# The scores of two heads in the two halves of TensorE's array, all heads of a chunk in one block

## The reference

```
for t in range(768):                       # for each batch and head
    m_new  = max(f[t] + m, i[t])
    f_s, i_s = exp(f[t] + m - m_new), exp(i[t] - m_new);  m = m_new
    C = f_s * C + i_s * outer(v[t], k[t])  # 40 x 40
    n = f_s * n + i_s * k[t]
    y[t] = sigmoid(o[t]) * (C @ q[t]) / max(|n @ q[t]|, 1)
x  = y, heads side by side                 # (2, 768, 320)
h  = relu(x @ w_in);  u, v = halves of h   # 512 columns each
x  = (u * (w_spatial @ normalised(v) + b)) @ w_out
xk, xr = mixes of x and x one token earlier
out = sigmoid(xr @ w_r) * (relu(xk @ w_k) ** 2 @ w_v)
```

## Time and profile before

| | |
|---|---|
| median of 3 runs | 311.3 us (309.66 to 312.32) |
| the profiled execution's own time | 309.62 us |
| its span, first to last instruction | 307.9 us |
| TensorE busy, matmuls | 297.3 us |
| VectorE, ScalarE, GpSimd busy | 208.1, 168.1, 68.8 us |
| mean granted clock of TensorE | 0.994 of full speed |

### The profile page before, as it was taken

How to read it: one execution, slowest core, us unless ns; L and a number is a source line. 1 busy time by engine, 2 the same in 40 slices (tenths; PEclk the granted TensorE clock), 3 DMA queues, 4 the chain that set the end, 5 groups by cost and what they waited for, 6 DMA issues and landing times.

```text
span 307.9 us, 5430 instructions
## 1 busy us (share of the span) xinstructions
PE 297.3 (97%) x1908; PEld 285.5 (93%) x1908; DVE 208.1 (68%) x443; ACT 168.1 (55%) x369; POOL 68.8 (22%) x92
## 2 busy tenths in 40 slices
PE   7998979999999999999999999999999999999996
PEld 3997969988999898899999999998999999999996
DVE  7986889979878779726424887878873377555111
ACT  5778796865546355513124676699682458255000
POOL 8325436324444413621111201400000000000000
PEclk9999997999999999999999999999999999999999
DMA  4959942554166054000060020320001000100011
GB/s 108 262 188 287 336 139 68 156 165 147 44 228 177 12 202 142 0 0 2 0 191 15 0 66 1 94 80 0 0 2 43 24 0 1 45 21 0 26 61 43
DMA packets 12778, 25.99 MB, mean 84 GB/s; under 512 B 2000, under 2 KB 5552, under 8 KB 12752
## 3 DMA queue, kind: packets, MB, share of 16 engines
q1 hardware_dynamic: 12752, 25.65, 26.5%
HBM read 23.63 MB, written 2.02 MB: 83 GB/s over the span
## 4 chain that ended last, share of the span: by engine, by line
PE 65%; DVE 13%; ACT 9%; issue 6%; DMA 3%; POOL 1%; DVEq 0%; SPq 0%; ACTq 0%; POOLq 0%
PE ps_e L1202 12%; PE ps_s L1202 10%; PE ps_v L1202 9%; PE ps_in L1202 6%; PE ps_out L1202 6%; PE ps_t L1202 6%; PE ps_z L1202 4%; PE ps_in L1282 4%; PE ps_s L1273 4%; PE ps_out L1292 2%; DVE shifted L1113 2%; DMA mb<-maxima 1%; DMA maxima<-mx 1%; PE ps_z L1301 1%; DVE mixb L1136 1%
## 5 line engine op out<-in xcount | busy, mean ns | idle before, releaser
L1273 PE MATMUL ps_s<-qkt 128*128 128x128 f32 x192 | 26.5, 282 | 0.2 <-DMA qkt<-in_qk 0.2
L1282 PEld LDWEIGHTS ps_in<-tok,pt 128*128 128x128 f32 x192 | 23.8, 192 | 2.6 <-issue 2.1
L628 ACT ACTIVATE et<-mb,gwt 128x128 f32<-128x128 f32 x80 | 25.4, 390 | 1.0 <-POOL mb L540 0.9
L1174 DVE TENSOR_TENSOR kr<-kr 128x384 f32<-128x384 f32 x32 | 17.7, 557 | 12.1 <-ACT kr L824 12.0
L1282 PE MATMUL ps_in<-tok,pt 128*128 128x42 f32 x192 | 24.4, 277 | 1.3 <-DVE num L937 1.3
L796 ACT ACTIVATE gh<-ut 128x384 fp32r<-128x384 f32 x16 | 8.4, 525 | 30.4 <-DVE ut L1140 30.4
L1273 PEld LDWEIGHTS ps_s<-qkt 128*128 128x128 f32 x192 | 24.0, 195 | 0.3 <-DMA qkt<-in_qk 0.3
L1202 PE MATMUL ps_v<-win,xth 128*128 128x512 f32 x60 | 20.7, 409 | 0.9 <-POOL win L553 0.8
L577 POOL TENSOR_TENSOR gl<-ut,gh 128x384 fp32r<-128x384 f32 x8 | 9.0, 1120 | 54.0 <-ACT gh L796 54.0
L900 DVE TENSOR_TENSOR pt<-ps_s,et 128x512 f32<-128x512 f32 x24 | 16.5, 689 | 6.5 <-PE ps_s L1273 2.6
L1202 PE MATMUL ps_e<-xth,win 128*128 128x384 f32 x60 | 18.0, 365 | 0.5 <-ACT ut L652 0.3
(11 more groups left out here) (307 smaller groups left out, 897.1 us busy)
## 6 DMA issues: line engine op xcount, KB each, us to landing
mb<-maxima SPq DMA_DIRECT2D x10, 512.0 KB, 5.8
tok<-in_vk SPq DMA_DIRECT2D x12, 328.0 KB, 4.6
qkt<-in_qk SPq DMA_DIRECT2D x24, 160.0 KB
sp_raw<-in_w_sp SPq DMA_DIRECT2D x6, 384.0 KB, 5.0
out_y<-ob SPq DMA_DIRECT2D x12, 160.0 KB, 1.7
wv_raw<-in_w_v SPq DMA_DIRECT2D x2, 640.0 KB, 4.9
win_raw<-in_w_in SPq DMA_DIRECT2D x4, 256.0 KB, 5.4
wk_raw<-in_w_k SPq DMA_DIRECT2D x2, 512.0 KB, 4.5
```

What stands on the lines that cost most here:

```text
L628: last = sc.activation(et[:, j, h, :], mb[u % 2][:, HH * j + h, :], ACT.Exp, bias=gwt[:, chunk(u), x:x + 1], scale=-1.0)
L1174: ve.tensor_tensor(kr[n % 4][:, :], kr[n % 4][:, :], kr[n % 4][:, :], ALU.mult).then_inc(sems["kk_done"], 1)
L1273: last = te.matmul(ps_s[j][:, h * CH:(h + 1) * CH], keys[u % NS][:, HH * j + h, :], queries[u % NS][:, h, :], start=True, stop=True)
L1282: last = te.matmul(p_in[:, HH * j + h, :], pt[:, j, h, :], vt[u % 2][:, HH * j + h, :], start=True, stop=True)
```

## The change

The keys are laid out like the queries: head g on partitions 0 to 39, head g + 4 on 64 to 103, in the same columns. A head's score matmul now reads its 40 partitions alone, one head in the upper and one in the lower half of the array, in turn, into the two banks. Both halves of a chunk's scores are one block, which stands in slot u behind `state(u-1)` and `values(u-1, 1)` and ahead of `carry(u-1)`; in slot 0 it stands ahead of `exponents(0, 1)`. It waits for `probs_done` 2u. The keys need no zeros, so that the fills of the places cover the queries alone.

```diff
-QK = (G + H) * CH
+QK = 2 * G * CH
+
+QS = 3 * G * CH
...
-    qkt = at("qkt", [KR, NS, QK], STK)
+    qkt = at("qkt", [KR, NS, QS], STK)
...
-    keys = [qkt[:, n, G * CH:QK].rearrange("p (h t) -> p h t", h=H) for n in range(NS)]
+    keys = [qkt[:, n, G * CH:QK].rearrange("p (g t) -> p g t", g=G) for n in range(NS)]
...
-                    sp.wait_ge(sems[f"pad{u}"], 2 if u == 0 else 1)
+                    sp.wait_ge(sems[f"pad{u}"], 1)
...
-                    parts = qkt[64 * r:64 * r + D, u % NS, :].rearrange("p (x t) -> p x t", x=3)
-                    sp.dma_start(parts[:, 0:r + 2:r + 1, :],
+                    parts = qkt[64 * r:64 * r + D, u % NS, 0:QK].rearrange("p (x t) -> p x t", x=2)
+                    sp.dma_start(parts,
...
-            gp.memset(qkt[:, 0, 0:QK // 2], 0.0).then_inc(sems["pad0"], 1)
...
-            gp.memset(qkt[:, 2, :], 0.0).then_inc(sems["pad2"], 1)
+            gp.memset(queries[2], 0.0).then_inc(sems["pad2"], 1)
...
-            sc.activation(qkt[:, 1, :].rearrange("p (x t) -> p x t", x=3),
-                          vr[:, :].unsqueeze(1).broadcast_to([KR, 3, HF]), ACT.Copy).then_inc(sems["pad1"], 1)
+            sc.activation(queries[1], vr[:, :].rearrange("p (g t) -> p g t", g=G),
+                          ACT.Copy).then_inc(sems["pad1"], 1)
...
-            ve.memset(qkt[:, 0, QK // 2:QK], 0.0).then_inc(sems["pad0"], 1)
+            ve.memset(queries[0], 0.0).then_inc(sems["pad0"], 1)
...
-            def scores(u, j):
+            def scores(u):
                 pe.wait_ge(sems[f"qk_in{u % NS}"], 32 * (u // NS + 1))
-                if u > 0 or j > 0:
-                    pe.wait_ge(sems["probs_done"], 2 * u + j - 1)
-                for h in range(HH):
-                    last = te.matmul(ps_s[j][:, h * CH:(h + 1) * CH], keys[u % NS][:, HH * j + h, :],
-                                     queries[u % NS][:, h, :], start=True, stop=True)
-                last.then_inc(sems["scores_mm"], 1)
+                pe.wait_ge(sems["probs_done"], 2 * u)
+                for g in range(G):
+                    for r in range(2):
+                        rows = slice(64 * r, 64 * r + D)
+                        last = te.matmul(ps_s[r][:, g * CH:(g + 1) * CH], keys[u % NS][rows, g, :],
+                                         queries[u % NS][rows, g, :], start=True, stop=True)
+                        if g == G - 1:
+                            last.then_inc(sems["scores_mm"], 1)
...
-                if u < NU:
-                    scores(u, 0)
+                if u == 0:
+                    scores(0)
...
                     values(u - 1, 1)
+                    if u < NU:
+                        scores(u)
...
-                if u < NU:
-                    scores(u, 1)
```

## The result

The changed kernel took 314.98 us, the median of four executions (314.67 to 318.14), against 310.91 us for the kernel before on the same chip (309.66 to 312.32): a ratio of 1.015, with a 95% interval of 1.010 to 1.020. It is slower; 311.1 us was forecast, with no change as the likeliest case. Its mean granted clock was 0.978, where before had 0.994.

A forecast was written before the change was run, and what follows sets the result against it. TensorE was taken as the bound from 45.5 to 62.3 and 75.7 to 114.9 us. Late start +2.0, clock +0.5, slot 5 -0.5, slots 8 to 11 -2.2 make -0.2: 311.1 us on the median, range 307.7 to 316.8.

The forecast's parts named there:

- the forecast of no change: Whole kernel: time the same within about 1%, 3.1 us; chance 0.45, against 0.18 faster and 0.37 slower.
- the clock: After slot 2's wait: idle TensorE may lower its granted clock, costing 0 to 0.8 us, taken as 0.5.
- about two such blocks: After slot 2's wait: scores, carry and transposes count as about two slowed score blocks, 0 to 0.8 us.
- The score block: A chunk's 16 score matmuls on TensorE: halves running at once take 1.27 us instead of 1.82.
- T: Length of a chunk's score block: 1.27 us (0.97 to 1.59) with halves at once; without, 1.82 to 2.33.
- both switches: Score block: two changes between whole and halved array a chunk, 0 to 0.31 us each, taken as 0.15.
- The rival of the loads one behind the other: Score block: loads do not run at once, 1.82 to 2.33 us with switches, nothing comes back; chance 0.38.
- The longer block that the prediction drew from that rule: Score block: if loads overlap matmuls only where the row group differs, the block would be longer than now.
- The late start: Slots 1 and 2: VectorE gets scores later, TensorE idles 3 us before spread_decay(2), x_high(0) starts 2.0 us late.
- that rival: Slots 2 to 4 absorb the lateness and the gain stays: -2.7 us, 308.0 us at the middle; chance 0.20.
- What comes back: Gains later: slot 5 0.5 us, slots 6 and 7 0, slots 8 to 11 four times 0.55, 2.2 us.
- The cover of VectorE: Slots 8 to 11: VectorE's numerators done at 5.3 us, TensorE wants them at 5.63; 0.3 us of cover.

The follow-up runs named there:

- place_alone: Kernel before, whole array and padded keys, with both score blocks moved behind state(u-1) and values(u-1, 1): 316.83 us, ratio 1.019.
- whole_first: Kernel before with both whole-array score blocks at the head of the slot: 313.04 us, ratio 1.008.
- early_halves: whole_first with the scores of chunks 0 to 3 alone by halves of the array: 319.79 us, ratio 1.020.
- block_first: Changed kernel with its halved scores block moved back to the head of each slot: 317.50 us, ratio 1.019.
- first_by_half: block_first with all four heads of one half first, then the four of the other: 320.97 us, ratio 1.029.
- late_behind: Kernel before up to slot 3; from chunk 4 on, halved scores in one block behind state(u-1) and values(u-1, 1): 309.57 us, ratio 0.997.
- filling: block_first with idle 512-column matmuls, results unread, added in slots 0 and 1: 312.78 us, ratio 1.000.
- halves_from_8: Kernel before with halved scores in one block at the head of the slot from chunk 8 on: 309.75 us, ratio 0.997.

## Why the prediction was wrong

The time lies in the range, the forecast of no change was wrong, and one term of the sum did most of it.

**The step that failed: the clock.** It was taken at 0.5 us, 0 to 0.8, from one case in the rows of before, where a score block was 0.37 us longer. Measured it is 4.0 us at ScalarE's table load: the 3.6 worked out above up to the transposes of x(0), and the transposes themselves at 0.85 instead of 0.49. With 4.0 in place of 0.5, and the other terms as written, the sum is +3.3 and the time 314.6 on the median, against 314.98. Three things were wrong in the step.

The price: the score block of the rows runs from 49.55 to 50.81, and the low stretch ends at 50.2. Half of that block stood at full clock already, so its 0.37 us is the price of half a block. Before's windows:

```profile
49.55:50.20 0.65, 0.65 (x5) 0.65 (x4) 0.65 (x2) 0.59 (x2) 0.57 (x2) 0.50 0.00 0
50.20:50.90 0.70, 0.70 (x8) 0.70 (x8) 0.48 (x2) 0.68 (x4) 0.58 (x2) 0.99 0.00 0
```

With nearly all of them in the low stretch, two whole-array blocks cost 3.49 - 1.82 = 1.7 us in place_alone, where "about two such blocks" were priced at 0.8 at most. The number: state and values behind the wait were left out, and in the changed kernel they took 1.50 and 1.64 us instead of 0.71 and 0.86 (chain at 21.12 and 22.62), although values moves only 42 columns. The length: the low stretch lasted 10 us, where the rows' case lasted 3.4 and place_alone's about as long. I had tied the fall to the wait alone and did not ask what the halves do to the clock. Whole_first against early_halves and block_first shows that halves in the first slots lower it; the low level lasted 20.5 us in block_first, where no wait over 0.41 us stood ahead.

**The score block.** T was taken at 1.27 us, 0.97 to 1.59; it is 1.09. The mechanism was right: sixteen instructions pass in 1.09 us, 0.068 each, where a whole array takes 0.11. I had put both switches, 0.3 us, into the block; some 0.12 (1.09 less the 0.97 worked out) lie in it, and 0.16 stand behind it, in the carry and the v product. The gain of a slot is 0.57 us, as forecast (0.55). The rival of the loads one behind the other, 1.72 us or more, is refuted. Its own sum was a little short: at T = 2.1 its terms make +5.3, not +5.0. The Trainium skill, TensorEngine Tiling (Array Packing), section Tiling Modes, says both that tiles load and multiply in parallel and that a change of mode drains TensorE; the trace agrees with the first, and leaves about 0.3 us to the second for the pair of switches, if the 0.97 is right. The Trainium skill, TensorE: Matmul & The Clock Gate, Part 3, has a load overlap a running matmul only where the row group differs; first_by_half agrees in part (1.64 us when neighbours share a half), while whole arrays overlap too. The longer block that the prediction drew from that rule didn't come: in turn, an instruction passes every 0.068 us, less than the 0.107 at which one load a time was priced.

**The late start.** Right: probabilities(1,0) ran at 15.68 (15.5 was worked out), the factors were copied at 20.24 (20.4), `spread_decay(2)` began at 20.51 (20.45). That T was 0.18 us less than taken didn't show in them: TensorE, done sooner with slot 0, waited 0.39 us for ScalarE, and the exponents of slot 1 began at 11.85 instead of 11.57. The idle time was forecast as one wait of 3 us and came as 0.40 and 1.82. That VectorE passes it on whole was right as well: nothing absorbed it, and that rival fell. On the way to values(4,0) it even grew, from 6.1 at the table load to 7.15; the timeline of VectorE has `normalise` at 2.11 us (42.75), where it was 1.05 (36.65 before), beside the same GpSimd work (below). place_alone has it at 2.03 us, so the halves aren't what doubles it. The counterpart is late_behind: with the first slots left alone the place costs nothing that can be measured.

**What comes back.** Slots 8 to 11: 2.2 forecast, 2.3 measured. Slots 5 to 7: 0.5 forecast, 0.5 measured. The cover of VectorE held in these slots, and was gone at their end: the last transposes waited 0.96 us for it (125.41), a wait that before doesn't have, and with it 1.0 us of the gain was lost; the sum had no term for that.

**The sum redone,** by the profiled executions: late start 2.1, clock 4.0, `normalise` 1.05, slots 5 to 7 -0.5, slots 8 to 11 -2.3, the tail +1.0: between 5.3 and 5.4, as measured. The medians differ by 4.1. That the sum with 4.0 alone comes so near the median is in part luck: it leaves out `normalise` and the tail, 2 us together.

What stays open: how the halves lower the clock, by the half array itself or by the shorter blocks and the waits that these open. For the second, TensorE was busy for 3.62 of 4.30 us ahead of block_first's fall, where whole_first had 4.30, and filling helped in some executions. Against it as the whole cause, first_by_half's block takes 1.64 us and its clock was as low, and in block_first the clock stayed at 0.50 for 20.5 us in which TensorE was never idle, while in place_alone the whole array had it back after some 3.4.

## What to carry over

Half the array in turn is a real gain for short contractions (sixteen 40-row score matmuls in 1.09 us instead of 1.8), but only where the granted clock stays up; read the clock of each stretch before and after, and try such blocks first in the stretch that TensorE bounds (halves_from_8 gained 1.2 us on before; early_halves lost 8.9, of which whole_first's place makes 2.1). Price a dip by all blocks that may fall in it, and take the price from a block that lies in the low stretch as a whole. And when a block moves behind others, follow the other engine's queue to the first thing that TensorE needs from it: here that is where the wait came up.

## What the hardware did that I had not expected

- Halves in turn in the first slots lower the mean clock: 0.947 to 0.978 in early_halves against 0.984 to 0.995 in whole_first.
- A busy TensorE doesn't always have its full clock: 20.50 of 20.50 us busy at a granted 0.50 in block_first.
- At the 1.2 GHz level blocks that move few columns take about double too: values (42 columns) 0.86 to 1.64, state (84) 0.71 to 1.50 us.
- Order decides the overlap: halves in turn 1.09 us, one half after the other 1.64, whole array 1.79.
- VectorE's `normalise` has no duration of its own. The changed kernel's timelines of VectorE and of GpSimd at the end of the recurrence:

```profile
120.67 2.04 DVE L975 TENSOR_SCALAR vnf<-vr,mv,rstd 128x512 f32<-128x512 f32 x1
```

```profile
120.60 1.83 POOL L549 TENSOR_TENSOR sp_lo<-sp_raw,sp_hi 128x768 fp32r<-128x768 f32 x1
```

In the changed kernel its instructions lasted 0.55 to 2.11 us, longest beside a GpSimd operation; before had such pairings with 1.23 and 1.47 us. What makes the difference was not tried.
